# Attention and two ReLU-like layers in f32: the first 256 tokens' attention rebuilt, and the values' matmuls on 64 weight columns

## The reference

```
keep = is_sink | in_window           # n_sink 4, window 128
a = softmax(where(keep, q @ k.T / 8, -1e9)); x = a @ v
h = x @ w_in  (512 x 2048);  g = piecewise(h): 0 below -1, (h+1)^2/4, h above 1
y = g @ w_out (2048 x 512)
h = y @ w_in2; g = where(h > 0, h, exp(min(h, 0)) - 1); out = g @ w_out2
```

## Time and profile before

| what | us |
|---|---|
| median of 3 runs | 666.1 (665.94 to 667.99) |
| profiled execution: its own time | 667.29 |
| profiled execution: span | 665.3 |
| TensorE busy | 642.4 |
| VectorE busy | 390.8 |
| ScalarE busy | 361.6 |
| alone phase ends, last x_lo read by TensorE | 40.5 |
| chunk 1, one pass of the first layer with attention beside it | 61.3 |

### The profile page before, as it was taken

The page is one execution under the profiler, slowest core; times in us unless marked ns, Lnnn a source line. Parts: engine busy times, 40 slices in busy tenths (PEclk is TensorE's granted clock), DMA queues, the critical chain, the costliest instruction groups (busy, mean ns, idle before and its releaser), DMA issues.

```text
span 665.3 us, 12399 instructions
## 1 busy us (share of the span) xinstructions
PE 642.4 (97%) x4204; PEld 582.4 (88%) x4204; DVE 390.8 (59%) x1022; ACT 361.6 (54%) x854; POOL 9.4 (1%) x28
## 2 busy tenths in 40 slices
PE   3888999999999999999999999999999999999998
PEld 3778999999999999999999998888888888888886
DVE  6989986886788588868866884322332222322221
ACT  6887766665665565656656665333453333533333
POOL 3000000000000000000000000000000000000000
PEclk9999999999999999999999999999999999999999
DMA  8477320431233023204205530000010000100001
GB/s 276 155 253 276 95 70 25 113 87 51 68 92 96 25 82 109 71 24 112 68 0 191 191 127 1 1 0 1 1 63 0 0 0 0 63 0 0 0 0 64
DMA packets 25805, 47.39 MB, mean 71 GB/s; under 512 B 2929, under 2 KB 10929, under 8 KB 25777
## 3 DMA queue, kind: packets, MB, share of 16 engines
q1 hardware_dynamic: 25776, 47.03, 22.7%
HBM read 43.88 MB, written 3.15 MB: 71 GB/s over the span
## 4 chain that ended last, share of the span: by engine, by line
PE 85%; DVE 11%; issue 2%; ACT 1%; DMA 1%; SPq 0%; ACTq 0%; DVEq 0%
PE h_ps L469 12%; PE h_ps L471 12%; PE h_ps L470 12%; PE y_ps L484 9%; PE y_ps L486 9%; PE y_ps L485 9%; PE s_ps L486 3%; PE s_ps L485 3%; PE s_ps L484 3%; PE o_ps L447 2%; PE t_ps L426 2%; PE s_ps L414 1%; DVE wout_lo L762 1%; PE s_ps L415 1%; PE o_ps L449 1%
## 5 line engine op out<-in xcount | busy, mean ns | idle before, releaser
L469 PE MATMUL h_ps<-x_hi,win_hi 128*128 128x256 f32 (+1 forms) x576 | 184.5, 320 | 1.3 <-DVE x_lo L769 0.5
L471 PE MATMUL h_ps<-x_hi,win_lo 128*128 128x256 f32 (+1 forms) x576 | 182.7, 317 | 0.0
L470 PE MATMUL h_ps<-x_lo,win_hi 128*128 128x256 f32 (+1 forms) x576 | 182.3, 316 | 0.0
L484 PE MATMUL y_ps<-g_hi,wout_hi 128*128 128x256 f32 (+1 forms) x480 | 145.2, 302 | 1.5 <-DVE g_lo L775 1.3
L486 PE MATMUL y_ps<-g_hi,wout_lo 128*128 128x256 f32 (+1 forms) x480 | 144.9, 302 | 0.0
L485 PE MATMUL y_ps<-g_lo,wout_hi 128*128 128x256 f32 (+1 forms) x480 | 144.6, 301 | 0.0
L792 DVE SCALAR_TENSOR_TENSOR g_full<-g_full,h_ps 128x512 f32<-128x512 f32 x48 | 33.0, 688 | 151.8 <-ACT g_full L622 151.8
L469 PEld LDWEIGHTS h_ps<-x_hi,win_hi 128*128 128x128 f32 x576 | 108.1, 188 | 11.1 <-DVE g_full L788 1.1
L470 PEld LDWEIGHTS h_ps<-x_lo,win_hi 128*128 128x128 f32 x576 | 108.2, 188 | 8.4
L471 PEld LDWEIGHTS h_ps<-x_hi,win_lo 128*128 128x128 f32 x576 | 108.2, 188 | 7.2
L775 DVE TENSOR_TENSOR g_lo<-g_full,g_hi 128x256 fp32r<-128x256 f32 (+1 forms) x144 | 73.6, 511 | 53.5 <-ACT g_hi L609 52.9
(11 more groups left out here) (122 smaller groups left out, 862.7 us busy)
## 6 DMA issues: line engine op xcount, KB each, us to landing
ks<-in_k SPq DMA_DIRECT2D x44, 260.0 KB, 2.7
vs<-in_v SPq DMA_DIRECT2D x24, 288.0 KB
qs<-in_q SPq DMA_DIRECT2D x44, 128.0 KB, 2.6
raw<-in_w_in SPq DMA_DIRECT2D x11, 512.0 KB, 4.6
raw<-in_w_out SPq DMA_DIRECT2D x11, 512.0 KB, 4.4
out_y<-xy SPq DMA_DIRECT2D x12, 256.0 KB, 2.1
xy<-in_w_in SPq DMA_DIRECT2D x5, 512.0 KB, 5.8
xy<-in_w_out SPq DMA_DIRECT2D x5, 512.0 KB, 6.3
```

The lines of the kernel that those rows point to most:

```text
L469: pe.matmul(o, win_hi[:, k, f], x_hi[:, k, :], start=(k == 0), stop=False)
L470: pe.matmul(o, win_hi[:, k, f], x_lo[:, k, :], start=False, stop=False)
L471: last = pe.matmul(o, win_lo[:, k, f], x_hi[:, k, :], start=False, stop=(k == KT - 1))
L484: pe.matmul(o, wout_hi[:, t, cols], g_hi[:, t % GR, :], start=begin, stop=False, skip_group_check=True)
```

## The change

The first 256 tokens' attention gets functions of its own. The keys seen by the two query blocks are 128 and 256 (384 columns a head), with no copy of the sinks; the sinks lie in the window. Queries and keys are not split: one f32 matmul a block, where the two heads of a pair lie on partitions 0 to 63 and 64 to 127 (two halves of TensorE's rows). Two pairs are in flight. Its values, and the values of all later chunks, use 64 weight columns a head, and the two heads' matmuls, which write the two halves of o_ps's partitions, alternate. Three weight pieces, not five, are split in the alone phase; the raw buffers used ahead of it are five, not four; loads are put in another order.

```
-SPLITS_ALONE = {6: [0], 7: [1], 8: [2], 9: [3, 4]}
+SPLITS_ALONE = {0: [0], 1: [1], 2: [2]}
...
+SEEN = P + WIN
+SEEN_OF = (slice(0, P), slice(P, SEEN))
+KEYS_OF = (slice(0, P), slice(0, WIN))
+IN_FLIGHT = 2
...
-        FEW = RAW - 2
+        FEW = RAW - 1
...
+            def first_scores_of(p):
+                pe.wait_ge(first_qk_loaded[p], 32)
+                (q, k), banks = first_qk[p], flight[p % IN_FLIGHT][0]
+                if p >= IN_FLIGHT:
+                    pe.wait_ge(first_exp, (p - IN_FLIGHT + 1) * 2 * QB)
+                for j in range(QB):
+                    for hh in range(2):
+                        dims = slice(HD * hh, HD * (hh + 1))
+                        last = pe.matmul(banks[hh][:, SEEN_OF[j]], q[dims, j * P:(j + 1) * P], k[dims, KEYS_OF[j]],
+                                         start=(j == 0), stop=True, skip_group_check=True)
+                last.then_inc(first_scores, 1)
...
-            def values(c, p, halves):
+            def values(c, p):
...
-                for hh in halves:
-                    v, pt = vs[:, s, :, HD * hh:HD * hh + P], probs_t[hh]
-                    pe.matmul(o_bank[:, 0:CT], v[:, 1, :], pt[:, P:P + CT], start=(hh == 0), stop=False, skip_group_check=True)
-                    pe.matmul(o_bank[:, 0:P], v[:, 0, :], pt[:, 0:P], start=False, stop=False, skip_group_check=True)
-                    pe.matmul(o_bank[:, P:CT], v[:, 2, :], pt[:, P + CT:P + CT + P], start=False, stop=False, skip_group_check=True)
+                for block, queries, keys_t in ((1, slice(0, CT), slice(P, P + CT)), (0, slice(0, P), slice(0, P)),
+                                               (2, slice(P, CT), slice(P + CT, 2 * CT))):
+                    for hh in range(2):
+                        dims = slice(HD * hh, HD * (hh + 1))
+                        pe.matmul(o_ps[dims, queries], vs[:, s, block, dims], probs_t[:, hh, keys_t],
+                                  start=(block == 1), stop=False, skip_group_check=True)
...
+            first_scores_of(0)
+            first_scores_of(1)
+            first_scores_of(2)
+            pe.wait_ge(ident_loaded, 16)
+            first_transposes(0)
+            first_scores_of(3)
+            first_values(0)
+            for p in range(1, PAIRS):
+                first_transposes(p)
+                first_values(p)
...
+            first_exponents(0)
+            first_exponents(1)
+            for p in range(PAIRS):
+                first_copies(p)
+                if p + IN_FLIGHT < PAIRS:
+                    first_exponents(p + IN_FLIGHT)
+                first_x(p)
+                for i in SPLITS_ALONE.get(p, []):
                     split_weights(i)
...
+            first_maxima(0)
+            first_maxima(1)
+            first_normalise(0)
+            first_maxima(2)
+            first_normalise(1)
+            first_maxima(3)
+            first_x(0)
+            first_normalise(2)
+            for i in SPLITS_ALONE[0]:
+                split_weights(i)
+            first_x(1)
+            for i in SPLITS_ALONE[1]:
+                split_weights(i)
+            first_normalise(3)
+            first_x(2)
+            for i in SPLITS_ALONE[2]:
+                split_weights(i)
+            first_x(3)
```

More of the change, by code:

```diff
@@ L191, in build @@
[L191 to L203, removed]
@@ L455, in values @@
+                pe.matmul(o_ps[:, 0:CT], vsink_parts[0:KS, :], sinks_t[0:KS, :], start=False, stop=True,
                           skip_group_check=True).then_inc(attn_ready, 1)
@@ L496, in layer_chunk @@
                     if attend is not None:
-                        for p, halves in BESIDE[3][t]:
-                            values(attend, p, halves)
+                        for p in BESIDE[3][t]:
+                            values(attend, p)
                         for h in BESIDE[2][t]:
@@ L504, in layer_chunk @@
                 outward(layer, c, FT - 1)
-            for t in range(len(ALONE[0])):
-                for h in ALONE[0][t]:
-                    scores(0, h)
-                for p, halves in ALONE[3][t]:
-                    values(0, p, halves)
-                if t == 2:
-                    pe.wait_ge(ident_loaded, 16)
-                for h in ALONE[2][t]:
-                    transposes(0, h)
+            first_scores_of(0)
[8 more added lines that the diff above has]
+                first_values(p)
             layer_chunk(0, 0, 1)
@@ new lines, in first_copies, with first_x @@
+            def first_copies(p):
+                probs_t = flight[p % IN_FLIGHT][3]
+                if p >= IN_FLIGHT:
+                    act.wait_ge(first_attn, p - IN_FLIGHT + 1)
+                for hh in range(2):
+                    act.wait_ge(first_probs_t, 2 * p + hh + 1)
+                    nc.scalar.copy(probs_t[hh][:, 0:SEEN], h_ps[hh][:, 0:SEEN]).then_inc(first_copied, 1)
+            def first_x(p):
+                act.wait_ge(first_attn, p + 1)
+                nc.scalar.copy(x_hi[:, p, :], flight[p % IN_FLIGHT][1][:, 0:CT]).then_inc(x_hi_ready, 1)
@@ L534, in split_head @@
-                nc.scalar.copy(q_parts, q).then_inc(qk_hi_ready, 1)
+                nc.scalar.copy(k_hi[:, :], ks[:, h % 2, :]).then_inc(qk_hi_ready, 1)
+                nc.scalar.copy(q_parts[:, :], qs[:, h % 2, :]).then_inc(qk_hi_ready, 1)
             def exponent(c, h):
                 p, hh = h // 2, h % 2
-                probs, banks = pair_work(c, p)[0], head_work(c, h)[3]
-                if hh == 0 and (not is_first(c) or p >= 2):
+                if hh == 0 and not begins(c, p):
                     act.wait_ge(probs_t_ready, pairs_before(c, p) * 2)
@@ L665, in _ @@
             nc.scalar.activation(t_ps[:, 0:1], half[:, :], ACT.Exp)
-            split_head(0, 0)
-            split_head(0, 1)
-            for t in range(len(ALONE[0])):
-                for h in ALONE[1][t]:
-                    exponent(0, h)
-                if t + 2 < HEADS:
-                    split_head(0, t + 2)
-                behind_layer(ALONE, 0, t)
-                for p, halves in ALONE[3][t]:
-                    if 1 in halves:
-                        split_x(0, 0, 0, [p])
-                for i in SPLITS_ALONE.get(t, []):
+            first_exponents(0)
[6 more added lines that the diff above has]
+                for i in SPLITS_ALONE.get(p, []):
                     split_weights(i)
@@ L816, in _ @@
             nc.vector.memset(sinks_t[:, :].bitcast(F32), 0.0).then_inc(zeros_set, 1)
-            split_head(0, 0)
-            for t in range(len(ALONE[0])):
-                if t + 1 < HEADS:
-                    split_head(0, t + 1)
-                for h in ALONE[0][t]:
-                    maxima(0, h)
-                for h in ALONE[1][t]:
-                    normalise(0, h)
-                for p, halves in ALONE[3][t]:
-                    if 1 in halves:
-                        split_x(0, 0, 0, [p])
-                for i in SPLITS_ALONE.get(t, []):
-                    split_weights(i)
-            dve.sem_inc(sinks_lo_ready, PAIRS)
+            first_maxima(0)
[16 more added lines that the diff above has]
+            first_x(3)
             split_head(1, 0)
```

336 lines of the change are left out of this document (198 added, 138 removed).

## The result

The changed kernel takes 658.6 us (median of 4 runs, 656.8 to 661.6) against 666.0 of the kernel before on the same chip: ratio 0.989, interval 0.984 to 0.994. I had forecast 646: the gain is 7.5 us where I had said 20, and 658.6 lies outside the 641 to 651 that I gave my own case (A). The profiled execution took 661.6 us, with a span of 659.9 against 665.3: 5.5 us less.

The account below looks back on a forecast made before the run. VectorE sets the time up to about 92 us, TensorE behind that. Terms -14.4 + 2.2 - 8.0 = -20.2 us against the profiled 667.3; with the runs' median at 666.1, forecast 646, range 641 to 659.

Parts of the forecast that it names:

- case (A): Values matmuls on the two column halves overlap: 646 us, own range 641 to 651; chance 0.58.
- Term 1: First attention: less VectorE work, so the last x_lo ends at 26.1 us instead of 40.51; -14.4 us.
- The walk through the four pairs: First attention, pairs timed in code order: x_lo ends at 15.9, 18.9, 22.3 and 25.3 us.
- Term 2: Chunk 0: two more splits +0.8, a stall for head 4's load +2.2, shorter values -0.8; sum +2.2 us.
- Term 3: Values beside the layer, chunks 1 to 4: overlapping column halves save 0.52 us a pair; -8.0 us in all.
- B: Column halves don't overlap, the f32 matmuls run one behind the other: 657.5 us; chance 0.22.
- C: Column halves overlap, with a drain at both ends or in part: 650 to 655 us; chance 0.09.
- D: Every change of column half drains the array, 1.1 us a pair, no overlap: about 678 us; chance 0.06.
- E: Start stays at 1.2 GHz and gains little, chunk 0's stall grows to 5 us, no overlap: about 664; chance 0.05.

Follow-up runs that it names:

- run 5: Changed kernel with head 4's loads ahead of the last weight piece and the activation tiles at their places in the kernel before; 646.6 us, ratio 0.971.
- Run 9: run 5 with one pair of heads in flight in the first attention instead of two; 660.1 us, ratio 0.990.
- run 3: Changed kernel with head 4's loads of chunk 1 issued ahead of the last weight piece instead of behind it; 655.8 us, ratio 0.984.
- 64-byte pair: Changed kernel with `small` 25 columns wide instead of 17, without and with head 4's loads moved ahead of the last weight piece; 654.8 and 653.4 us.
- run 6: Kernel before with only the values beside the layer (chunks 1 to 5) on 64 weight columns a head, heads in turn; 658.8 us, ratio 0.989.
- run 7: run 5 with head 0's three values windows beside the layer ahead of head 1's, instead of the heads in turn; 655.5 us, ratio 0.985.
- run 12: TensorE alone, no other engine at work, the layers' matmul groups at 26 places of the moving operand; 512-column slots 226.8 to 234.1 ns.
- 13: TensorE alone, weights moved as well as moving parts, and the 256-column form entered in twelve ways; 226.7 to 234.3 ns, and 117.8 ns for 256 columns.
- 8: run 5 with head 0's two matmuls ahead of head 1's in the first attention's scores and values; 645.9 us, ratio 0.968.
- run 15: Changed kernel with the tiles at their places in the kernel before and its own order of loads; 648.2 us, ratio 0.972.
- 11: run 5 with every activation tile 256 bytes behind its place in the kernel before; 646.3 us, ratio 0.967.
- run 1: Changed kernel with `small` 25 columns wide instead of 17, moving every tile behind it by 32 bytes; 654.8 us, ratio 0.983.

## Why the prediction was wrong, step by step

**Term 1 (-14.4) was right.** The last x_lo ends 13.7 us earlier after the change and 14.9 in run 5, which lacks the slow stretch of the start. The walk through the four pairs held: in run 5 x_lo ends at 15.8, 19.4, 22.8 and 25.6 us, where I had 15.9, 18.9, 22.3 and 25.3. The scores' overlap is there too: pair 1's eight records start between 4.94 and 5.80 us in run 5 and fill 1.3 us at the 1.2 GHz level, where I had 1.7 with overlap and 2.6 in series. Run 9 shows that the second pair in flight is needed for the gain: without it 13.4 of the 14.9 us are gone. The kernel before had several heads under way too, so what fewer columns, the missing splits of keys and queries and the two weight splits less are worth by themselves was not tried.

**Term 2 (+2.2) had the right mechanism and half the size.** The step was "It lands 4 to 6 us behind the split: a stall of 2 to 4 us", of which I took 2.2. The wait was 3.27 us, inside that range, but I had not counted what TensorE does behind it: 27 matmuls in 5 us, where run 3 has 40. Chunk 0 is 6.4 us longer than before; moving one load takes back 4.6 (3.6 at the places of before, 2.7 in the 64-byte pair). The two more splits less the shorter values are then 0.9 with the places right, where I had 0.

**Term 3 (-8.0) was right to 1 us.** By itself (run 6) it is -7.1 in chunks 1 to 4. The block is 1.02 us, where I had 1.08, and going in costs 0.09, where I took 0.08. That the 1.08 came so near is in part luck: I had the two halves start 0.1 to 0.2 us apart, and beside the layer they start 0.01 apart, so they overlap almost wholly. The saving of a pair is 0.44 us, not 0.52. The Trainium skill (TensorEngine Tiling (Array Packing), Key Properties) says that changing the tiling mode drains TensorE; a change at both ends costs 0.11 us here, and the 0.32 that I had worked out for a drain did not come. The Trainium skill (TensorE: Matmul & The Clock Gate, Part 3: Packing small matmuls) says that column tiles run at once; the traces agree, 12 records in 1.02 us, as long as the halves follow one another in turn (1.50 us in run 7).

**The step that failed is one that I did not write: the sum gives the unchanged matmuls their old price.** Some 3,400 of them run in the changed kernel on tiles that stand 32 bytes further, because `small` grew by 8 columns. That is 9.1 us by the medians of runs 3 and 5 and 8.9 by their stages behind chunk 0, of which 5.1 in the second layer, which the change does not touch. Add it to the stall: 646 + 4.6 - 2.2 + 9.1 = 657.5, against 658.6 measured; with the stall at 2.8 us, its price by the medians, it is 655.7. With both mended the kernel takes 646.6. The sum without its stall gives 643.8; of the 2.8 us between, term 3 is 0.9 and the two more splits 0.9, and term 1 is 0.5 the other way.

**The rivals.** B gave 657.5, close to what came, and was wrong in all it said: the halves overlap, and chunk 1 takes 60.3 us, not 61.5. C and D fell with the block of 1.01 us. Of E, the stall's price of 4.6 us came near its 5; its slow start did not come, though 6.8 us of the start did run at 1.2 GHz. A time near a rival's is no evidence for the rival; the stages are.

The Trainium skill (SBUF — State Buffer, Operand start alignment) asks only that an operand start at a multiple of its element size, and says that this is about legality, not speed. All places here keep that rule, and their speeds differ by 3% (226.7 to 233.4 ns).

## What to carry to other kernels

Before pricing an edit, compare the addresses of all tiles, not only the instructions: a small tile that grows moves everything behind it, and here that cost 9 us, more than the new values gained (7.1). When a stage whose code is the same takes another time, count its instructions in a fixed window of both traces; a full TensorE with fewer matmuls at the same granted clock points to its operands' places. Price a stall that TensorE sees with the passes at half clock behind it, and write matmuls of two column halves in turn.

## What the runs showed of the hardware

- The slot of a 512-column fp32r matmul depends on the place of the moving operand against that of the weights within 256 bytes: 226.7 ns at a difference of 0, 228.9 at 64, 232.4 at 128 (233.4 in run 12), 233.3 at 192, and 233.3 to 234.3 where one or both places are 32 off a multiple of 64. No other engine need be at work.
- With the 256-column form beside attention the order was another: chunks 1 to 4 took 58.4 us each at a difference of 192, 59.5 at 64, 59.9 at 128, 60.1 at 0 and 60.2 at 96, with the values' matmuls in turn. Kernels with the same difference agree to 0.1 us. Why the order is not that of the 512-column form stays open; the two paces of the next point may have a part in it.
- The same first-layer code at the same places has two paces: 113 ns or 118 (run 12 against 13; chunk 5 took 44.9 us in runs 7, 8, 9 and 15, and 46.2 in runs 5, 6 and 11). What chooses between them stays open. In chunk 5 it moves a kernel's time by 1.3 us.
- f32 matmuls on the two column halves start 0.00 to 0.04 us apart, and a matmul can start ahead of one of the other half that is written before it (run 7). Twelve records take 1.02 us in turn, 1.50 with one head behind the other, 1.68 on 128 columns.
- In chunk 0, TensorE's granted clock fell to 0.5 around the end of a wait of TensorE: for 6.8 us with a wait of 3.6 us (the changed kernel), but for 3.4 us with one of 4.3 (run 15) and one of 3.2 (run 1). The length of the slow stretch doesn't follow that of the wait.
